# Softmax sums and reciprocals in two parts, with three changes of order in the layers after attention

## The chip, the cores and the metric

The kernel runs on one core of a Trainium2 chip. The metric is the device time of one execution in microseconds (us); the shown time is the median of three runs. All matrix products are made in fp32 accuracy: each operand is split into a high and a low part of type fp32r, and a product is three matmuls (high by high, high by low, low by high).

## The reference

Three layers follow each other. The first is attention in which a query sees only the keys with the same 6 sign bits (a hash by a random projection):

```python
def _attn_ref(q, k, v, proj):                       # q, k, v: 2 x 8 x 768 x 64
    q_bits = (einsum('bhsd,dk->bhsk', q, proj) > 0)  # proj: 64 x 6; k_bits the same
    mask = q_bucket[:, :, :, None] == k_bucket[:, :, None, :]
    scores = where(mask, scale * q @ k.T, -1e9)
    attn = exp(scores - max(scores))
    attn = attn / (sum(attn) + 1e-09)
    return attn @ v
def _moe_ref(x, w_gate, w_val, w_out):              # 1536 x 512 -> 1536 -> 512
    return (sigmoid(x @ w_gate) * (x @ w_val)) @ w_out
def _moe2_ref(x, w_in, w_out):                      # 1536 x 512 -> 2048 -> 512
    h = x @ w_in
    return where(h >= 1, h, where(h <= -1, 0, (h + 1) ** 2 / 4)) @ w_out
```

## The kernel before

The kernel is written by hand: one program for each engine, and semaphores between them. Each engine runs its own program strictly in order, so a wait holds up everything behind it on that engine.

**Attention** takes 96 steps g: 16 heads, and 6 blocks of 128 queries in each. Two heads make a pair i (g // 12), and u (g % 12) is the place in the pair. Three blocks make a half j (g // 3). A step has these pieces. TensorE (PE) makes the scores of block g (`scores`, L752 and L755). VectorE (DVE) reads them out of PSUM with the row minimum (`evacuate`, L1274). ScalarE (ACT) makes the exponential and its row sum (`exponential`, L979). GpSimd (POOL) multiplies the row by the reciprocal of its sum (`normalise`, L539). Five steps later PE transposes the probabilities (`turn_probs`, L764), ACT copies the high part (`high_probs`, L975), DVE makes the low part (`low_probs`, L1285), and PE multiplies by the values (`weigh`, L784 and L785).

Sums and reciprocals go by halves. POOL adds 1e-9 to three sums at once (`sums`, L534), DVE takes three reciprocals (`reciprocals`, L1279), and then POOL normalises the three blocks. In POOL's program stand between these: the splitting of the values of the next head in two instructions (`split_v`, L519 and L521) at u = 2 and u = 8, the sum of two output parts (`add_half`, L647), and in pairs 1 to 6, at u = 11, one part of the first weight set of the next layer (`first_set`, L552 to L559 and L588, L589).

PSUM has three double banks for scores, transposed probabilities and transposed inputs in turn: the use that comes three uses later may start only when the earlier one has been read out. For turn_probs(n) that is evacuate(n + 4). For scores(g) it is low_probs(g - 7), except where a transposition of queries or keys lies between; then it can be evacuate(g - 1). All engines count the same steps g. DVE's step is: hash bits (at two places of a pair), evacuate(g), reciprocals (every third step), low_probs(g - 5), low part of transposed queries or keys (at two places of a pair).

**The layers after attention** are 40 sets n of weights (24 for gate and value in turn, 16 for the last layer). They are multiplied by a scheme with 7 products for 8 blocks (`product(n, r)`, L806 to L808, 6 matmuls each), and the sums are formed while the products are read out of PSUM. ACT empties product 0 of a set (L1054) and DVE the six others (`empty`, L1342 and L1349). A product goes to one of the banks that `banks_for` names, and waits until what was last in that bank has been emptied. Sets 0, 12, 24 and 32 (`FIRSTS`) begin a new group of rows. Between products PE makes units of the output projection (`down`, L841 to L859); `units(n, r)` says how many after each product. On DVE, `value_set` multiplies the gates in: `gate_quarter` (L1362), `gate_second` (L1368) and `gate_first` (L1373). POOL forms sums of the weights and their low parts all the time (L552 to L577).

## Time and profile before

| | |
|---|---|
| median of 3 runs | 787.28 us (787.16 to 787.37) |
| the profiled execution | 787.15 us, its span 785.4 us |
| PE busy | 772.0 us, 98% of the span |
| DVE, ACT, POOL busy | 563.7, 461.1, 539.1 us |
| granted clock of PE, mean | 0.998 of full speed |

The trace is of one execution. A row of the timeline gives start, duration, engine, source line, operation, output<-inputs and the count of instructions that were put together; in brackets stands how long the engine was idle before it and what ended that. The starts of matmuls are measured and their ends are modelled; two matmuls of 384 columns that follow each other without a wait start 0.17 us apart.

### The profile page before, as it was taken

How to read it: one execution, taken by the hardware profiler on the slowest of the kernel's cores; microseconds unless marked ns; L12 is line 12 of the kernel's file. 1: busy time of each engine (PE TensorE's matmuls, PEld its weight loads, DVE VectorE, ACT ScalarE, POOL GpSimd, SP SyncE). 2: the span in 40 equal slices, each digit the busy share in tenths (PEclk: the TensorE clock that was granted, in tenths of full speed). 3: DMA queues.
4: the chain of work that ended last, by engine and by line, in shares of the span. 5: the costliest groups of instructions: out<-in, count | busy, mean ns of one | idle time of the engine just before them, and what ended most of it. 6: DMA issues, size and time to landing. Idle time of an engine off the chain costs nothing.

```text
span 785.4 us, 12212 instructions
## 1 busy us (share of the span) xinstructions
PE 772.0 (98%) x4403; PEld 717.3 (91%) x4403; DVE 563.7 (72%) x869; ACT 461.1 (59%) x731; POOL 539.1 (69%) x533
## 2 busy tenths in 40 slices
PE   7999999999999899999999999999999999999998
PEld 6899999999989899999899999999899988999996
DVE  6888888889888655665764666676777776756654
ACT  4889989989997442443463343356555475644433
POOL 4568667788889968877596877736957755565420
PEclk9999999999999999999999999999999999999999
DMA  7784675474300222122021221120121011201002
GB/s 153 181 189 107 164 164 114 101 165 108 92 1 12 71 81 75 34 81 81 28 82 55 67 68 40 68 81 28 56 80 54 29 52 52 84 28 53 1 1 81
DMA packets 61931, 60.09 MB, mean 77 GB/s; under 512 B 28384, under 2 KB 51632, under 8 KB 61872
## 3 DMA queue, kind: packets, MB, share of 16 engines
q1 hardware_dynamic: 61712, 59.32, 28.4%
q8 instruction: 35, 0.57, 0.3%
q14 instruction: 24, 0.20, 0.1%
q10 hardware_dynamic: 160, 0.00, 0.0%
HBM read 37.75 MB, written 3.15 MB: 52 GB/s over the span
## 4 chain that ended last, share of the span: by engine, by line
PE 86%; DVE 5%; ACT 4%; issue 3%; POOL 2%; DMA 0%; SPq 0%; DVEq 0%; POOLq 0%; ACTq 0%
PE ps L806 12%; PE ps L807 12%; PE ps L808 12%; PE ps L845 9%; PE ps L764 6%; PE ps L859 6%; PE ps L858 6%; PE ps L857 6%; PE ps L846 4%; PE ps L784 3%; PE ps L785 3%; PE ps L752 3%; PE ps L755 3%; ACT ph L975 1%; PE ps L713 1%
## 5 line engine op out<-in xcount | busy, mean ns | idle before, releaser
L806 PE MATMUL ps<-xop,wset 128*128 128x384 f32 x560 | 189.9, 339 | 2.6 <-DVE u L1349 2.1
L807 PE MATMUL ps<-xop,wset 128*128 128x384 f32 x560 | 189.1, 338 | 0.0
L808 PE MATMUL ps<-xop,wset 128*128 128x384 f32 x560 | 188.6, 337 | 0.0
L1349 DVE TENSOR_TENSOR u<-ps,u 128x384 f32<-128x384 f32 x144 | 79.7, 553 | 103.4 <-PE ps L808 102.6
L564 POOL TENSOR_TENSOR wset<-stage,wset 128x512 fp32r<-128x512 f32 x39 | 57.8, 1482 | 108.0 <-ACT wset L1022 108.0
L806 PEld LDWEIGHTS ps<-xop,wset 128*128 128x128 f32 x560 | 105.3, 188 | 13.1 <-DVE u L1349 3.2
L1285 DVE TENSOR_TENSOR pl<-ps,ph 128x768 fp32r<-128x768 f32 x96 | 91.6, 956 | 24.2 <-ACT ph L975 23.2
L807 PEld LDWEIGHTS ps<-xop,wset 128*128 128x128 f32 x560 | 105.4, 188 | 3.6
L539 POOL TENSOR_SCALAR probs<-probs,small 128x768 f32<-128x768 f32 x96 | 88.8, 932 | 24.6 <-DVE small L1279 21.9
L808 PEld LDWEIGHTS ps<-xop,wset 128*128 128x128 f32 x560 | 105.2, 188 | 0.0
L979 ACT ACTIVATE probs<-probs,small 128x768 f32<-128x768 f32 x96 | 90.0, 937 | 7.5 <-DVE probs L1274 6.9
L570 POOL TENSOR_TENSOR wset<-wsum,wset 128x1024 fp32r<-128x1024 f32 x39 | 94.3, 2418 | 0.0
L1274 DVE TENSOR_SCALAR_CACHE_REDUCE probs<-ps 128x768 f32<-128x768 f32 x96 | 90.9, 950 | 1.7 <-PE ps L755 1.1
L975 ACT CAST ph<-ps 128x768 fp32r<-128x768 f32 x96 | 76.8, 801 | 19.6 <-PE ps L764 17.8
L764 PE MATMUL ps<-ident,probs 128*128 128x128 f32 x576 | 79.0, 273 | 1.8 <-DVE probs L1274 1.6
L845 PE MATMUL ps<-hh,wo 128*128 128x512 f32 x192 | 75.5, 398 | 0.0
L764 PEld LDWEIGHTS ps<-ident,probs 128*128 128x128 f32 x576 | 67.3, 140 | 8.9 <-POOL probs L539 3.1
L859 PE MATMUL ps<-wo,hl 128*128 128x512 f32 x192 | 75.2, 392 | 0.0
L858 PE MATMUL ps<-wo,hh 128*128 128x512 f32 x192 | 75.2, 392 | 0.0
L857 PE MATMUL ps<-wo,hh 128*128 128x512 f32 x192 | 74.8, 389 | 0.0
L784 PE MATMUL ps<-ph,v 128*128 128x384 f32 x192 | 72.2, 376 | 0.1
L1054 ACT COPY u<-ps 128x384 f32<-128x384 f32 x40 | 19.1, 478 | 89.7 <-PE ps L808 89.6
(135 smaller groups left out, 1696.1 us busy)
## 6 DMA issues: line engine op xcount, KB each, us to landing
stage<-in_moe_w_in_dram SPq DMA_DIRECT2D x16, 512.0 KB, 3.9
stage<-in_moe_w_out_dram SPq DMA_DIRECT2D x14, 512.0 KB, 3.7
stage<-in_moe_w_gate_dram SPq DMA_DIRECT2D x12, 512.0 KB, 4.3
stage<-in_moe_w_val_dram SPq DMA_DIRECT2D x12, 512.0 KB, 3.6
ops<-qh SPq DMA_DIRECT2D x15, 384.0 KB, 5.2
ops<-kh SPq DMA_DIRECT2D x28, 192.0 KB, 3.4
qn<-in_q_dram SPq DMA_DIRECT2D x16, 192.0 KB, 4.5
kn<-in_k_dram SPq DMA_DIRECT2D x16, 192.0 KB, 4.3
```

The lines of the kernel that those rows point to most:

```text
L570: pool.tensor_tensor(weights(n, 1)[:, 3:7], wsum[:, :], weights(n, 0)[:, 3:7].bitcast(F32), ALU.subtract).then_inc(w_split, 1)
L764: last = pe.transpose(dst[:, t * P:(t + 1) * P], probs[n % RING][:, t * P:(t + 1) * P], ident[:, :])
L784: pe.matmul(o_bank(j), v2[h % 2][:, t, :], ph[j % 2][:, t, :], start=(t == 0), stop=False)
L806: pe.matmul(dst, high[:, c, :], high_x(r)[:, c, :], start=(c == 0), stop=False)
L807: pe.matmul(dst, high[:, c, :], low_x(r)[:, c, :], start=False, stop=False)
L808: last = pe.matmul(dst, low[:, c, :], high_x(r)[:, c, :], start=False, stop=(c == 1))
L845: pe.matmul(main, w[:, cols], h[:, t % 3, 0:512], start=(first and n == 0), stop=(last_tile and n == 2))
L857: pe.matmul(ps[:, r, :], hh[:, t % 3, rows], wh, start=first, stop=False)
L858: pe.matmul(ps[:, r, :], hh[:, t % 3, rows], wl, start=False, stop=False)
L859: last = pe.matmul(ps[:, r, :], hl[:, t % 3, rows], wh, start=False, stop=last_tile)
L1274: dve.tensor_scalar(probs[g % RING].rearrange("p (s n) -> p s n", s=2), score_slot(g), NO_MATCH, None, ALU.min, ALU.min, accum_out=lowest( ...
L1285: dve.tensor_tensor(pl[j % 2][:, :, cols], turned_slot("T", n).rearrange("p (t n) -> p t n", t=T), ph[j % 2][:, :, cols].bitcast(F32), ALU ...
```

## The change

Four things are changed.

1. Each half's sums and reciprocals are taken in two parts: blocks 0 and 1 of the half together (part 0), block 2 alone (part 1). POOL takes part 0 at its step g = 3j + 2 and part 1 at g = 3j + 3, and normalises block g - 2 instead of g - 3. DVE takes the reciprocals of part 0 at step 3j + 2 and of part 1 at 3j + 3, and behind low_probs instead of ahead of it.
2. The query bits of pair 1 are made at u = 7 instead of u = 6.
3. In sets 1 and 13, `gate_quarter` stands behind `empty(n, 2)` instead of behind `empty(n, 4)`.
4. Sets 25 and 33 have four banks instead of two for their first four products. In sets 11 and 23, one unit of the output projection is made after product 5 (11 instead of 12 are left for after product 6).

```diff
--- before.py
+++ after.py
@@ -159,7 +159,7 @@
             return (3, 6)[kind == "K"] if i else (5, 6)[kind == "K"]
 
         def bits_at(i, kind):
-            return signs_at(i, kind) + 1
+            return signs_at(i, kind) + 1 if i else 7
 
         uses = [("Q", 0), ("K", 0)]
         for g in range(STEPS):
@@ -228,6 +228,8 @@
             if n < 2:
                 return (4, 5, 2, 3) if n else (4, 5, 2) if r == R - 1 else (4, 5)
             if n in FIRSTS and r == R - 1 or n == FIRSTS[1] + 1 or n in (2, FIRSTS[1] + 2) and r < 2:
+                return (6, 7, 2, 3)
+            if n in (FIRSTS[2] + 1, FIRSTS[3] + 1) and r < 4:
                 return (6, 7, 2, 3)
             return (6, 7)
 
@@ -529,13 +531,14 @@
                     pool.wait_ge(coded[(i - 1) % 2][1], all_coded(i - 1, 1))
                 pool.tensor_scalar(codes[:, :], bits[:, :], mscale, 1.0, ALU.mult, ALU.mult).then_inc(z_codes, 1)
 
-            def sums(j):
-                pool.wait_ge(exp_done, HT * j + HT)
-                pool.tensor_scalar(total(HT * j, HT), total(HT * j, HT), EPS, 1.0, ALU.add,
-                                   ALU.mult).then_inc(sums_done, 1)
+            def sums(j, part):
+
+                n, m = HT * j + 2 * part, 2 - part
+                pool.wait_ge(exp_done, n + m)
+                pool.tensor_scalar(total(n, m), total(n, m), EPS, 1.0, ALU.add, ALU.mult).then_inc(sums_done, 1)
 
             def normalise(n):
-                pool.wait_ge(rcp_done, n // HT + 1)
+                pool.wait_ge(rcp_done, 2 * (n // HT) + 1 + n % HT // 2)
                 pool.tensor_scalar(probs[n % RING][:, :], probs[n % RING][:, :], rcp(n), 1.0, ALU.mult,
                                    ALU.mult).then_inc(normed, 1)
 
@@ -659,14 +662,16 @@
                     pool.wait_ge(z_codes, 1)
                 pool.tensor_copy(dst, src[D:P, :].bitcast(F32)).then_inc(second_keys, 1)
                 pool.wait_ge(second_keys, n + 1)
-            for g in range(STEPS + HT):
+            for g in range(STEPS + 2):
                 i, u = g // U, g % U
+                if g % HT == 2:
+                    sums(g // HT, 0)
                 if g % HT == 0 and g:
-                    sums(g // HT - 1)
-                if g >= HT:
-                    normalise(g - HT)
+                    sums(g // HT - 1, 1)
+                if g >= 2:
+                    normalise(g - 2)
                 if g % HT == 0 and 12 <= g < STEPS:
-                    add_half((g - 12) // HT, g - HT + 1)
+                    add_half((g - 12) // HT, g - 1)
                 if g < STEPS and g % T == 2:
                     split_v(g // T)
                 if u == bits_at(i, "K") and i < NP - 1:
@@ -882,7 +887,7 @@
                     return 0
                 if n < N1:
                     if ends:
-                        return 3 * KT if r == R - 1 else 0
+                        return {R - 2: 1, R - 1: 3 * KT - 1}.get(r, 0)
                     return int(r > 2 if n % 2 == 0 else r in (0, 1, 2, 4))
                 if ends:
                     return (2, 2, 1, 1, 1, 1, 20)[r]
@@ -1274,9 +1279,10 @@
                 dve.tensor_scalar(probs[g % RING].rearrange("p (s n) -> p s n", s=2), score_slot(g), NO_MATCH, None,
                                   ALU.min, ALU.min, accum_out=lowest(g)).then_inc(evacuated, 1)
 
-            def reciprocals(j):
-                dve.wait_ge(sums_done, j + 1)
-                dve.reciprocal(rcp(HT * j, HT), total(HT * j, HT)).then_inc(rcp_done, 1)
+            def reciprocals(j, part):
+                n, m = HT * j + 2 * part, 2 - part
+                dve.wait_ge(sums_done, 2 * j + part + 1)
+                dve.reciprocal(rcp(n, m), total(n, m)).then_inc(rcp_done, 1)
 
             def low_probs(n):
                 j = n // HT
@@ -1409,12 +1415,11 @@
                 t, g = 2 * pair_of(n), group_of(n) + 1
                 empty(n, 1)
                 empty(n, 2)
-                alone = n - 1 in FIRSTS or n + 1 in FIRSTS
-                if not alone:
+                if n + 1 not in FIRSTS:
                     gate_quarter(n)
                 empty(n, 3)
                 empty(n, 4)
-                if alone:
+                if n + 1 in FIRSTS:
 
                     gate_quarter(n)
                 empty(n, 5)
@@ -1490,10 +1495,12 @@
                 if u == bits_at(i, "K") and i < NP - 1:
                     make_bits(i + 1, True)
                 evacuate(g)
-                if g % HT == 0 and g:
-                    reciprocals(g // HT - 1)
                 if g >= LAG:
                     low_probs(g - LAG)
+                if g % HT == 2:
+                    reciprocals(g // HT, 0)
+                if g % HT == 0 and g:
+                    reciprocals(g // HT - 1, 1)
                 if i == NP - 1 and u in (4, 5):
                     rest_x(0, u - 4)
                 if u == turn_at(i, "Q") and i < NP - 1:
@@ -1501,7 +1508,7 @@
                 if u == turn_at(i, "K") and i < NP - 1:
                     low_turned("K", i + 1)
             rest_x(0, 4)
-            reciprocals(2 * NH - 1)
+            reciprocals(2 * NH - 1, 1)
             low_probs(STEPS - 5)
             low_probs(STEPS - 4)
             add_last(2 * NH - 3)
```

The source lines of the changed kernel are shifted by 2 to 6. In the order of instructions below, brackets name the semaphores that an instruction waits for.

POOL around steps 32 and 33 (u = 8 and 9 of a pair), the kernel before: L534 is `sums`, L539 `normalise`, L519 and L521 `split_v`, L647 `add_half`.

```order
L539 TENSOR_SCALAR probs<-probs,small 128x768 [waits rcp_done]
L519 CAST v<-vn 128x6x64 [waits o_ready,v_in0]
L521 TENSOR_TENSOR v<-vn,v 128x6x64 [waits v_high]
L534 TENSOR_SCALAR small<-small 128x3 [waits exp_done]
L539 TENSOR_SCALAR probs<-probs,small 128x768 [waits rcp_done]
L647 TENSOR_TENSOR x<-x,o_part 64x384 [waits o_copied,normed]
L539 TENSOR_SCALAR probs<-probs,small 128x768 [waits rcp_done,o_done]
L539 TENSOR_SCALAR probs<-probs,small 128x768 [waits rcp_done]
```

The same stretch of a pair in the changed kernel: `sums` is L538 there, `normalise` L542, `split_v` L521 and L523.

```order
L538 TENSOR_SCALAR small<-small 128x2 [waits exp_done]
L542 TENSOR_SCALAR probs<-probs,small 128x768 [waits rcp_done]
L521 CAST v<-vn 128x6x64 [waits o_ready,v_in1]
L523 TENSOR_TENSOR v<-vn,v 128x6x64 [waits v_high]
L538 TENSOR_SCALAR small<-small 128x1 [waits exp_done]
L542 TENSOR_SCALAR probs<-probs,small 128x768 [waits rcp_done]
L650 TENSOR_TENSOR x<-x,o_part 64x384 [waits o_copied,normed]
L542 TENSOR_SCALAR probs<-probs,small 128x768 [waits rcp_done,o_done]
```

The two instructions of `split_v` stood ahead of the sums of three blocks; now they stand between the two parts, behind the normalisation of the half's first block.

DVE over three steps of a pair, the kernel before: L1274 is `evacuate`, L1279 `reciprocals`, L1285 `low_probs`.

```order
L1274 TENSOR_SCALAR probs,small<-ps 128x768 [waits pt_ready,scores_ready]
L1285 TENSOR_TENSOR pl<-ps,ph 128x6x128 [waits pt_high]
L1274 TENSOR_SCALAR probs,small<-ps 128x768 [waits pt_ready,scores_ready]
L1279 RECIPROCAL small<-small 128x3 [waits sums_done]
L1285 TENSOR_TENSOR pl<-ps,ph 128x6x128 [waits pt_high]
L1274 TENSOR_SCALAR probs,small<-ps 128x768 [waits pt_ready,scores_ready]
```

And in the changed kernel, with `evacuate` at L1279, `reciprocals` at L1285 and `low_probs` at L1291:

```order
L1279 TENSOR_SCALAR probs,small<-ps 128x768 [waits pt_ready,scores_ready]
L1291 TENSOR_TENSOR pl<-ps,ph 128x6x128 [waits pt_high]
L1285 RECIPROCAL small<-small 128x2 [waits sums_done]
L1279 TENSOR_SCALAR probs,small<-ps 128x768 [waits pt_ready,scores_ready]
L1291 TENSOR_TENSOR pl<-ps,ph 128x6x128 [waits pt_high]
L1285 RECIPROCAL small<-small 128x1 [waits sums_done]
```

There are now two reciprocals, one behind each of two successive steps of DVE, and each waits for its own sums.

## Rows read from the trace of the kernel before

**Rows 1.** Page, part 1: busy time of each engine, share of the span, instructions.
```profile
PE 772.0 (98%) x4403; PEld 717.3 (91%) x4403; DVE 563.7 (72%) x869; ACT 461.1 (59%) x731; POOL 539.1 (69%) x533
```

**Rows 2.** Windows: stretch and length; busy time of PE, PEld, DVE, ACT, POOL; granted clock; DMA.
```profile
210.00:260.00 50.00, 48.64 (x299) 44.70 (x299) 41.34 (x71) 40.89 (x69) 44.20 (x48) 1.00 0.07 22
267.30:270.60 3.30, 3.30 (x11) 2.51 (x11) 2.25 (x4) 0.90 (x1) 3.22 (x3) 0.51 0.69 245
```

**Rows 3.** Timeline, DVE, steps 32 to 34 (start, duration, line, operation, idle before).
```profile
88.35 0.95 DVE L1274 TENSOR_SCALAR_CACHE_REDUCE probs<-ps 128x768 f32<-128x768 f32 x1
...
89.22 0.17 DVE L1279 RECIPROCAL small<-small 128x3 f32<-128x3 f32 x1
89.72 0.96 DVE L1285 TENSOR_TENSOR pl<-ps,ph 128x768 fp32r<-128x768 f32 x1 [0.33 <-ACT ph L975]
90.60 0.95 DVE L1274 TENSOR_SCALAR_CACHE_REDUCE probs<-ps 128x768 f32<-128x768 f32 x1
```

**Rows 4.** Timeline, POOL, a split of the values and what follows, without idle.
```profile
216.26 0.49 POOL L519 CAST v<-vn 128x384 fp32r<-128x384 f32 x1
216.84 1.01 POOL L521 TENSOR_TENSOR v<-vn,v 128x384 fp32r<-128x384 f32 x1
217.94 0.20 POOL L534 TENSOR_SCALAR small<-small 128x3 f32<-128x3 f32 x1
218.44 0.91 POOL L539 TENSOR_SCALAR probs<-probs,small 128x768 f32<-128x768 f32 x1 [0.30 <-DVE small L1279]
```

**Rows 5.** Timeline, DVE, the reciprocal between the last two rows above.
```profile
218.18 0.18 DVE L1279 RECIPROCAL small<-small 128x3 f32<-128x3 f32 x1
```

**Rows 6.** Timeline, PE, transposition of block 30 in step 35 (u = 11).
```profile
91.89 0.82 PE L764 MATMUL ps<-ident,probs 128*128 128x128 f32 x6
```

**Rows 7.** Timeline, DVE, steps 27 and 28 (u = 3 and 4).
```profile
73.12 0.95 DVE L1274 TENSOR_SCALAR_CACHE_REDUCE probs<-ps 128x768 f32<-128x768 f32 x1
...
74.22 0.96 DVE L1285 TENSOR_TENSOR pl<-ps,ph 128x768 fp32r<-128x768 f32 x1
...
75.75 0.96 DVE L1274 TENSOR_SCALAR_CACHE_REDUCE probs<-ps 128x768 f32<-128x768 f32 x1
```

**Rows 8.** Timeline, PE, scores of step 29 (u = 5).
```profile
77.56 0.51 PE L752 MATMUL ps<-ops 128*128 128x384 f32 x2
```

**Rows 9.** Timeline, POOL, the first part of the first weight set (u = 11, pair 1).
```profile
64.59 0.74 POOL L552 TENSOR_TENSOR wsum<-stage 128x256 f32<-128x256 f32 x1
...
66.81 0.20 POOL L534 TENSOR_SCALAR small<-small 128x3 f32<-128x3 f32 x1
```

**Rows 10.** Timeline, DVE, evacuations of steps 24 and 25 (u = 0 and 1).
```profile
66.07 0.95 DVE L1274 TENSOR_SCALAR_CACHE_REDUCE probs<-ps 128x768 f32<-128x768 f32 x1
...
68.06 0.95 DVE L1274 TENSOR_SCALAR_CACHE_REDUCE probs<-ps 128x768 f32<-128x768 f32 x1
```

**Rows 11.** Timeline, DVE, set 1's first gating, and the emptying that PE waits for.
```profile
259.97 2.10 DVE L1362 TENSOR_TENSOR hid<-hid,u 128x384 f32<-128x384 f32 x1
...
265.71 0.56 DVE L1349 TENSOR_TENSOR u<-ps,u 128x384 f32<-128x384 f32 x1
```

**Rows 12.** Timeline, POOL, weight set 2 beside it.
```profile
257.31 1.29 POOL L564 TENSOR_TENSOR wset<-stage,wset 128x512 fp32r<-128x512 f32 x1
...
259.25 2.41 POOL L570 TENSOR_TENSOR wset<-wsum,wset 128x1024 fp32r<-128x1024 f32 x1
```

**Rows 13.** Timeline, PE, product 3 of set 2.
```profile
266.33 0.44 PE L806 MATMUL ps<-xop,wset 128*128 128x384 f32 x1 [2.13 <-DVE u L1349]
```

**Rows 14.** Timeline, PE, sets 11 and 33: last matmul before a short gap, first behind it.
```profile
376.46 0.34 PE L808 MATMUL ps<-xop,wset 128*128 128x384 f32 x1
376.87 0.44 PE L806 MATMUL ps<-xop,wset 128*128 128x384 f32 x1
...
665.85 0.34 PE L808 MATMUL ps<-xop,wset 128*128 128x384 f32 x1
666.41 0.44 PE L806 MATMUL ps<-xop,wset 128*128 128x384 f32 x1 [0.22 <-ACT u L1054]
```

## The prediction

> **What bounds the kernel now.** I read the page's first part first: PE is busy 98% of the span [rows 1], so little can be won, and anything that holds PE up is paid in full. The windows say where PE still waits. Between 210 and 260 us, the last pair of heads and the change to the next layer, it is busy 48.64 of 50 us, and in a stretch of 3.3 us behind the largest wait its granted clock is 0.51 of full speed, the lower of its two levels, 1.2 GHz [rows 2]. Then I read the timelines of DVE and PE side by side, because in attention DVE follows PE closely. The reader is to see that nothing separates the instructions of DVE at steps 33 and 34: low_probs starts at 89.72 and lasts some 0.87 us to the next start, and evacuate(34) starts at 90.60 at once [rows 3]. That evacuation lasts about 0.95 us with the read of its accumulator, and PE can start about 0.15 us later, so turn_probs(30) could start at 91.71. It starts at 91.89 [rows 6]. DVE has 0.18 us to spare there.
>
> **Part 1, the sums and reciprocals.** What it removes is nothing: the same three blocks are summed, inverted and normalised. What it adds are 32 more sums of 0.20 us on POOL and 32 more reciprocals, of which each holds DVE for 0.09 us. What it moves is the point: the reciprocal of part 1 waits on DVE for a sum that POOL makes only after it has normalised the first block, and after that block has waited for part 0's reciprocal, which DVE makes one step earlier. So between two successive steps of DVE, POOL now has a chain of its own, and what is queued behind the waiting reciprocal on DVE is evacuate(3j + 4), for which PE and ACT wait.
>
> The price of that chain comes from POOL's rows. From a reciprocal to the normalisation behind it pass 0.26 us, from a sum to the reciprocal 0.24 us, a split of the values lasts 0.58 + 1.10 us to the sum behind it, and a normalisation 0.87 us [rows 4, 5]. From DVE's one reciprocal to the end of its next (0.09 us) the chain is 0.27 + 0.87 + 1.69 + 0.24 + 0.09 = 3.16 us with a split, 1.47 us without one, and 3.7 us with the 2.22 us of the first weight set's first part [rows 9].
>
> At u = 8 DVE reaches part 0's reciprocal at 88.35 and would reach part 1's at 90.60, 2.25 us later [rows 3]. It must wait until 91.51: evacuate(34) is 0.91 us late, and with 0.18 us to spare turn_probs(30) is 0.73 us late. The six middle pairs (1 to 6) have this pattern with 0.70 to 0.75 us; pair 0 gives 0.34 and pair 7 0.58 by the same working. Together 4.4 + 0.9 = **5.3 us**.
>
> At u = 2 part 0 is at 73.12, and low_probs ends at 75.09, where the hash bits follow and then, at 75.75, evacuate(28) [rows 7]. The chain ends at 76.28, and bits and evacuation are 1.18 us late. The scores of step 29 wait for that evacuation; they start at 77.56 [rows 8], 0.70 us after it would let them (75.75 + 1.11 = 76.86). The stall is 0.47 us, six times, and 0.44 in pair 7, which is 3.3 us. In pair 0 part 1 holds up the low part of the keys and all that follows until step 7. No row shows this wait; its bounds are 0, if the values' split is done in time, and the chain's full delay of 1.2 us. I take 0.9, nearer to the upper end, since DVE does not wait for PE in those steps. Together **4.2 us**.
>
> At u = 11 of pairs 1 to 6 a part of the first weight set stands in the place of the split: 1.3 to 2.25 us, the longest in pair 1 [rows 9]. There evacuate(25) started at 68.06 and part 0 is at 66.07 [rows 10]; the chain ends at 69.79, the delay is 1.73 us, the reserve 0.50 us and the stall 1.24 us. The other five give 0.34, 0.93, 0.47, 0.99 and 0.51. Together **4.5 us**. At u = 5 nothing stands on POOL between the parts; 1.47 us is less than DVE's own two instructions, and the cost is nothing. If POOL came late there, it would cost what u = 8 does.
>
> What part 1 gives: blocks are normalised up to one step earlier. In the steady pairs turn_probs starts where the evacuation lets it, 0.18 us later, and not where POOL lets it [rows 3, 6], so that is worth nothing. In the last pair and at the start PE waits for evacuations and not for POOL, and I take nothing for it there either; the most it could give is a part of the 1.4 us that PE idles between 210 and 260 us [rows 2].
>
> **Part 2, the query bits.** They are 0.5 us of DVE moved from ahead of evacuate(6) to ahead of evacuate(7), for which turn_probs(3) waits at once. The work ahead of evacuate(7) stays the same, so it gives nothing.
>
> **Part 3, the gating.** In set 1 gate_quarter takes 2.10 us instead of some 0.5, and ends when POOL's L570 has ended and half a microsecond more has passed: 259.97 + 2.10 = 262.07 against 259.25 + 2.41 = 261.66 [rows 11, 12]. Placed behind empty(n, 2), it would be reached at 257.5, inside L564, which ends at 258.6 [rows 12], and be done at 259.0. But the products in between are emptied by 261.0, and then gate_second, with two inputs in SBUF as well, comes before POOL's long L570 is over, which by now is 0.45 us later itself. It would run from 262.1, the last gating would be done near 264.7, and the empty(2, 1) that PE waits for starts at 264.8 instead of 265.71 [rows 11]. The wait of 2.13 us [rows 13] shrinks by **0.85 us**. The Trainium skill (SBUF — State Buffer, Who interferes with whom) says that a DVE instruction with two SBUF inputs and a GpSimd instruction that reads SBUF shut each other out for the whole instruction and don't share the time; by this rule the moved gate only hands the block on to the next one. If they shared the bandwidth, the move would give up to 1.5 us, and the sum below would be 0.65 us lower. The trace agrees with the rule: the 2.10 us end 0.41 us after L570.
> In set 13 the same move ends PE's short wait for the first hidden tile, 0.45 us. The clock: PE ran at the lower level for 3.3 us [rows 2] from about 1 us after its wait; that cost 1.7 us. Whether 1.3 us of waiting does it too no row tells; I leave the 1.7 us in, and put them into the range.
>
> **Part 4, banks and units.** The gaps before products in sets 11 and 33 are 0.24 and 0.38 us over the regular 0.17, with 0.11 us more behind each [rows 14]; sets 23 and 25 have the like, 0.34 and 0.39 us. All four waits are for a bank, and go. The unit that moves is PE work moved to where PE waited; what it covered after product 6 has 11 units left. Together **1.6 us**.
>
> **The sum.** 5.3 + 4.2 + 4.5 = 14.0 us are lost, 0.85 + 0.45 + 1.6 = 2.9 us are won: 11.1 us more than the profiled execution's 787.15 us (0.13 below the median of the three), and so 798.2 us.
>
> **The rivals.** *POOL is in time.* If DVE in the new order reaches part 1's reciprocal 3.2 us after part 0's and not 2.25, nothing waits, and what is left are parts 3 and 4: 787.3 - 2.9 = 784.4 us, or 782.7 us if the clock stays up. This is the faster side. It decides at u = 8: whether the two steps of DVE are longer than POOL's chain. For it speaks that DVE is idle 0.33 and more before low_probs [rows 3], so it has air in some steps; against it, that this idle time is already in the 2.25 us.
> *Half is absorbed.* A late DVE need not hold PE if PE is late itself: once the pair has lost its 0.7 us at u = 8, the stalls at u = 11 and u = 2 may find more reserve. Then only u = 8, the start and half of the rest count: 5.3 + 0.9 + 3.9 - 2.9 = 7.2, and less if u = 2 goes wholly: 791 to 794.5 us.
> *The delays go through whole.* DVE is busy without a gap at u = 8 to 11, and ACT with it. If the reserves are gone after the first delay, each costs its full length: 6.8 at u = 8, 8.4 at u = 2 and the start, 7.0 at u = 11, less 2.9: 19 us more, 806 us.
> *The change doesn't do what it says:* the blocks are normalised earlier, and no instruction of PE starts earlier for it. This is part of my forecast, not against it.
>
> **Chances.** The forecast (794.5 to 802 us) 0.58, half absorbed (789 to 794.5) 0.15, whole delays (802 to 807) 0.13, POOL in time 0.10, and 0.04 that gains and losses meet near zero. The range of 8 in 10 leaves out the faster case and the far end of the whole delays: 790.5 to 804 us. Faster by over 0.2% (1.6 us, about what a measurement of this kernel can tell from no change) 0.09, within it 0.04, slower 0.87.
>
> **What would show it.** In the changed kernel DVE's reciprocals have 20 or so waits for POOL's sums of 0.5 to 1.7 us, at u = 3, 9 and 0 of the pairs; PE's waits for evacuations by DVE grow from under 2 us to over 8; the last pair ends near 254 instead of 240 us. PE's wait in set 2 is 1.3 us instead of 2.13, and those in sets 11, 23, 25 and 33 are gone. I am wrong if the reciprocals of part 1 run without idle time before them, or if they wait and the transpositions behind don't move.

## The result, and the profile after

The changed kernel takes **799.5 us** (median of 4 runs, 799.2 to 799.9), the kernel before 787.22 us beside it (785.75 to 787.37): 1.0161 times as long, with a 95% interval of 1.0147 to 1.0175. Slower was forecast, 798.2 us in a range of 790.5 to 804.0. The profiled execution took 799.71 us, its span is 797.6 us, 12.2 us more than before.

The page of the changed kernel, its part 1 and, below, the shares of the chain that ended last:

```profile
PE 776.8 (97%) x4403; PEld 716.1 (90%) x4403; DVE 564.5 (71%) x901; ACT 462.2 (58%) x731; POOL 544.0 (68%) x565
```

```profile
PE 76%; POOL 7%; issue 7%; DVE 6%; ACT 3%; DMA 0%; SPq 0%; POOLq 0%; DVEq 0%; ACTq 0%
```

DVE's busy time grew by 0.8 us for 32 more reciprocals, POOL's by 4.9 us for 32 more sums (compare [rows 1]); no work that was added explains 12 us. The chain now runs 7% of its length through POOL, an engine that is idle for a third of the time. The waits of the changed kernel show how (engine, what waits, line, releaser; us in all, times, longest):

```profile
POOL probs L542 <- DVE small L1285: 44.7, 32, 2.2
...
DVE small L1285 <- POOL small L538: 19.2, 24, 1.5
...
PE ps L769 <- DVE probs L1279: 6.8, 12, 1.2
...
PE ps L757 <- DVE probs L1279: 2.0, 3, 0.9
```

L1285 is `reciprocals`, L538 `sums`, L542 `normalise`, L1279 `evacuate`; L769 is the transposition `turn_probs` and L757 `scores`. POOL waits for DVE's reciprocal and DVE for POOL's sum, in turn: each engine has air, and neither can use it. The row for the wait of DVE's reciprocals was 1.5 us in 4 waits before, and it is 19.2 us in 24 waits now. The third and fourth rows are what PE pays of it.

Now one place in full, u = 8 of pair 2, where [rows 3] and [rows 6] stood before. Timeline of DVE in the changed kernel:

```profile
93.42 0.15 DVE L1285 RECIPROCAL small<-small 128x2 f32<-128x2 f32 x1
93.49 0.94 DVE L1279 TENSOR_SCALAR_CACHE_REDUCE probs<-ps 128x768 f32<-128x768 f32 x1
...
94.79 0.96 DVE L1291 TENSOR_TENSOR pl<-ps,ph 128x768 fp32r<-128x768 f32 x1 [0.36 <-ACT ph L980]
96.44 0.16 DVE L1285 RECIPROCAL small<-small 128x1 f32<-128x1 f32 x1 [0.69 <-POOL small L538]
96.54 0.96 DVE L1279 TENSOR_SCALAR_CACHE_REDUCE probs<-ps 128x768 f32<-128x768 f32 x1
```

Timeline of POOL beside it, which does without a gap what DVE waits for:

```profile
93.67 0.91 POOL L542 TENSOR_SCALAR probs<-probs,small 128x768 f32<-128x768 f32 x1 [2.19 <-DVE small L1285]
94.52 0.50 POOL L521 CAST v<-vn 128x384 fp32r<-128x384 f32 x1
95.11 1.02 POOL L523 TENSOR_TENSOR v<-vn,v 128x384 fp32r<-128x384 f32 x1
96.22 0.19 POOL L538 TENSOR_SCALAR small<-small 128x1 f32<-128x1 f32 x1
```

And PE, the scores of step 35 and the transposition of block 30, which waits for evacuate(34):

```profile
96.26 0.51 PE L757 MATMUL ps<-ops 128*128 128x384 f32 x2
...
97.65 0.84 PE L769 MATMUL ps<-ident,probs 128*128 128x128 f32 x6 [0.54 <-DVE probs L1279]
```

From the one reciprocal to the end of the next pass 96.44 + 0.09 - 93.42 = 3.11 us. DVE's own work between them would have ended 0.69 us earlier. The transposition starts 1.39 us after the scores, where it was 0.69 us before: 0.70 us lost. In the other middle pairs (1 to 6) it is 0.66 to 0.71 us at this place, and 0.12 to 0.13 us more at the first scores of the next pair.

The table gives the length of each pair (from its first scores to the next pair's, the last one to the transposition of block 95), from the starts in the traces of the kernel before, the changed one, and three experiments that are told below:

| pair | before | changed | lost | part 1 alone (e1) | split later (e3) | both later (e4) |
|---|---|---|---|---|---|---|
| 0 | 23.17 | 24.56 | 1.39 | 25.47 | 23.21 | 23.23 |
| 1 | 28.65 | 30.02 | 1.37 | 30.04 | 28.67 | 28.62 |
| 2 | 28.74 | 31.20 | 2.46 | 31.24 | 30.21 | 28.87 |
| 3 | 28.76 | 30.40 | 1.64 | 30.40 | 29.43 | 28.85 |
| 4 | 28.79 | 30.71 | 1.92 | 30.72 | 29.75 | 28.87 |
| 5 | 28.79 | 30.36 | 1.57 | 30.43 | 29.42 | 28.86 |
| 6 | 28.77 | 30.94 | 2.17 | 30.92 | 29.95 | 28.86 |
| 7 | 37.09 | 39.36 | 2.27 | 39.41 | 39.99 | 39.03 |

Attention lost 14.8 us. The layers behind it won 3.3 us. The first scores came at 13.47 instead of 12.80 us, 0.7 us later, and the three make the 12.2 us. This start varies: over all traces of this case it lies between 12.79 and 14.58 us. PE's first transpositions, in the kernel before and in the changed one:

```profile
5.10 0.88 PE L713 MATMUL ps<-ident,qn 128*128 128x128 f32 x6 [0.38 <-DMA qn<-in_q_dram]
```

```profile
5.07 1.54 PE L718 MATMUL ps<-ident,qn 128*128 128x128 f32 x6 [0.30 <-DMA qn<-in_q_dram]
```

The queries were there as early as before; the six transpositions took 1.54 us instead of 0.88, with a granted clock of 1.00 shown in both traces. Why is open. In e3 and e9 below, which have part 1 too, the scores start at 12.99 and 13.18 us. So the 0.7 us are not put down to the change.

Behind attention PE's large wait ahead of product 3 of set 2 has become short. Timeline of PE (before: [rows 13]), and of the gating and POOL's L573 ahead of it (before: [rows 11, 12]), in the changed kernel:

```profile
280.62 0.45 PE L811 MATMUL ps<-xop,wset 128*128 128x384 f32 x1 [0.72 <-DVE u L1355]
```

```profile
273.09 1.44 DVE L1368 TENSOR_TENSOR hid<-hid,u 128x384 f32<-128x384 f32 x1
...
276.62 1.68 DVE L1374 TENSOR_TENSOR hid<-hid,tmp 128x768 f32<-128x768 f32 x1
```

```profile
275.08 2.40 POOL L573 TENSOR_TENSOR wset<-wsum,wset 128x1024 fp32r<-128x1024 f32 x1
```

The wait is 0.72 us instead of 2.13, and the granted clock did not fall behind it.

### The profile page after: what moved, and what is told of

Same layout as the page of the kernel before. It is cut to its first block, busy times and chain, and to the rows that moved or that the text cites. A ratio compares the mean times of both kernels' runs of the same rounds, so it can differ in the third digit from the quotient of the medians.

```text
span 797.6 us, 12278 instructions
## 1 busy us (share of the span) xinstructions
PE 776.8 (97%) x4403; PEld 716.1 (90%) x4403; DVE 564.5 (71%) x901; ACT 462.2 (58%) x731; POOL 544.0 (68%) x565
## 4 chain that ended last, share of the span: by engine, by line
PE 76%; POOL 7%; issue 7%; DVE 6%; ACT 3%; DMA 0%; SPq 0%; POOLq 0%; DVEq 0%; ACTq 0%
PE ps L811 11%; PE ps L812 11%; PE ps L813 11%; PE ps L850 8%; PE ps L862 6%; PE ps L864 6%; PE ps L863 6%; PE ps L851 4%; PE ps L769 4%; POOL probs L542 3%; PE ps L757 2%; PE ps L760 2%; PE ps L789 2%; PE ps L790 1%; ACT ph L980 1%
## 5 line engine op out<-in xcount | busy, mean ns | idle before, releaser
L542 POOL TENSOR_SCALAR probs<-probs,small 128x768 f32<-128x768 f32 x96 | 88.9, 927 | 50.3 <-DVE small L1285 44.7
L1291 DVE TENSOR_TENSOR pl<-ps,ph 128x768 fp32r<-128x768 f32 x96 | 91.6, 955 | 21.4 <-ACT ph L980 19.1
L573 POOL TENSOR_TENSOR wset<-wsum,wset 128x1024 fp32r<-128x1024 f32 x39 | 94.3, 2417 | 0.0
L1279 DVE TENSOR_SCALAR_CACHE_REDUCE probs<-ps 128x768 f32<-128x768 f32 x96 | 90.7, 947 | 1.3 <-PE ps L760 1.1
L769 PE MATMUL ps<-ident,probs 128*128 128x128 f32 x576 | 79.3, 274 | 8.7 <-DVE probs L1279 6.8
L769 PEld LDWEIGHTS ps<-ident,probs 128*128 128x128 f32 x576 | 66.1, 140 | 19.6 <-POOL probs L542 11.9
L1355 DVE TENSOR_TENSOR hid<-ps,u 128x384 f32<-128x384 f32 x84 | 46.5, 554 | 35.4 <-PE ps L813 33.8
```

Of the source, the lines that this page charges most:

```text
L542: pool.tensor_scalar(probs[n % RING][:, :], probs[n % RING][:, :], rcp(n), 1.0, ALU.mult, ALU.mult).then_inc(normed, 1)
L573: pool.tensor_tensor(weights(n, 1)[:, 3:7], wsum[:, :], weights(n, 0)[:, 3:7].bitcast(F32), ALU.subtract).then_inc(w_split, 1)
L769: last = pe.transpose(dst[:, t * P:(t + 1) * P], probs[n % RING][:, t * P:(t + 1) * P], ident[:, :])
L1291: dve.tensor_tensor(pl[j % 2][:, :, cols], turned_slot("T", n).rearrange("p (t n) -> p t n", t=T), ph[j % 2][:, :, cols].bitcast(F32), ALU ...
L1355: dve.tensor_tensor(dst, bank(n, r), other, ALU.add).then_inc(e_dve, 1)
```

## The experiments

The first question was whether part 1 alone makes the loss, and whether the rest is worth what was said.

**e1_parts_alone** is the kernel before with part 1 and nothing else.

> The kernel before with part 1 of the change alone (sums and reciprocals of each half in two parts), the other three parts undone. Theory (the reciprocal of part 1 waits on DVE for a sum that stands behind the split of the values or a part of the first weight set on POOL): all of the loss is here, 14 to 15 us, so 801 to 802.5 us. Rival (the loss of 12.3 us is shared between attention and the changes behind it, some of which cost): below 799.5 us.

Measured: 803.0 us (802.47 to 803.78), 1.0198 [1.0179, 1.0218]. The pairs from 1 on are as long as in the changed kernel (table), and the waits are the same:

```profile
DVE small L1283 <- POOL small L536: 19.4, 24, 1.5
```

That is 15.6 us more than the kernel before beside it (787.45), 0.5 us above the forecast of 801 to 802.5. So the whole loss is part 1's. Pair 0 is 0.9 us longer than in the changed kernel. That has a cause of its own: with part 1, PE waits at the start twice for about 1 us (before the change once), and in this trace (windows: stretch, length, busy PE, PEld, DVE, ACT, POOL, clock) the clock fell behind it, while in the changed kernel's it did not:

```profile
22.50:26.00 3.50, 3.50 (x16) 3.47 (x15) 2.43 (x6) 2.53 (x5) 0.94 (x2) 0.59 1.08 219
```

```profile
22.50:26.00 3.50, 3.50 (x25) 3.46 (x24) 2.60 (x7) 3.28 (x6) 0.74 (x3) 1.00 1.07 224
```

In the same stretch PE issued 16 matmuls at 0.59 of full speed, and 25 in the changed kernel. The mean clock was 0.998 in all four runs of e1, and 1.0 in all four of the changed kernel.

**e2_without_parts** is the changed kernel without part 1, so parts 2 to 4 on the kernel before.

> The changed kernel with part 1 undone: only the gating, the banks and units and the query bits are changed. Theory: 3.3 us less than before (set 2's wait and the stretch at the lower clock behind it go, and four short waits for banks), 783.9 us. Rival (the clock's stretch went by chance of the run, and only waits are won): 2 us less or fewer, 785.3 us or more.

Measured: 783.99 us (783.88 to 785.57), 0.9961 [0.9948, 0.9973]: 3.5 us less than the kernel before beside it (787.45), and the fastest kernel of this study. Its attention is as long as before (232.69 us to block 95, 232.76 before). The gains behind attention are real and stand beside part 1's loss; they don't come from it.

The second question was what in part 1 costs the time. The theory names POOL's instructions between the two parts. Their place can be changed without taking any work away.

**e3_split_later**: the values are split one step later, behind the second sum.

```diff
                     sums(g // HT - 1, 1)
+                if g < STEPS and g % T == 3:
+                    split_v(g // T)
                 if g >= 2:
                     normalise(g - 2)
...
-                if g < STEPS and g % T == 2:
-                    split_v(g // T)
```

> The changed kernel with one thing moved on POOL: the split of the values stands right behind the sum of part 1 (at u = 3 and 9) instead of ahead of it (u = 2 and 8). Same instructions, same number of waits. Theory: the waits at the start, at u = 3 and at u = 9 go, 9.5 us of the loss, so 790 us; what is left are the parts of the first weight set, 4.5 us. Rival (the many small instructions and round trips between POOL and DVE cost the time wherever the split stands): 797 to 800 us.

Measured: 792.46 us (791.98 to 792.69), 1.0063 [1.0045, 1.0081], 7.0 us less than the changed kernel; 9.5 us less had been expected, so the size was missed. Pair 1, whose only POOL work between parts was the split, is back at 28.67 us. Pairs 2 to 6 are still too long by 1.47, 0.67, 0.96, 0.63 and 1.18 us, which follow the lengths of the first weight set's parts in the order that the forecast had (1.24, 0.34, 0.93, 0.47 and 0.99), 0.03 to 0.33 us larger. And the last pair is 2.90 us too long, more than in the changed kernel. The place, in step 24 of this kernel, POOL and then DVE:

```profile
66.64 0.91 POOL L542 TENSOR_SCALAR probs<-probs,small 128x768 f32<-128x768 f32 x1 [0.41 <-DVE small L1285]
67.51 0.74 POOL L555 TENSOR_TENSOR wsum<-stage 128x256 f32<-128x256 f32 x1
68.21 0.74 POOL L556 TENSOR_TENSOR wsum<-stage 128x256 f32<-128x256 f32 x1
68.89 0.74 POOL L558 TENSOR_TENSOR wsum<-wsum,stage 128x256 f32<-128x256 f32 x1
69.72 0.19 POOL L538 TENSOR_SCALAR small<-small 128x1 f32<-128x1 f32 x1
```

```profile
66.39 0.15 DVE L1285 RECIPROCAL small<-small 128x2 f32<-128x2 f32 x1
...
69.95 0.16 DVE L1285 RECIPROCAL small<-small 128x1 f32<-128x1 f32 x1 [1.49 <-POOL small L538]
```

From part 0 to the end of part 1 pass 3.65 us; 3.7 had been worked out.

**e4_both_moved**: besides, the first weight set's parts stand at u = 0 of the next pair, behind the second sum.

```diff
+                if u == 0 and 2 <= i < 8:
+                    first_set(i - 2)
...
-                if 1 <= i < 7 and u == 11:
-                    first_set(i - 1)
```

> As the run before, and the parts of the first weight set stand behind the sum of part 1 too (u = 0 of the next pair instead of u = 11). Theory: no reciprocal waits long for POOL any more, another 4.5 us go, 785 to 786 us, within 2 us of the kernel without part 1. Rival (round trips): 796 us or more.

Measured: 787.16 us (786.75 to 788.94), 0.9999 [0.9987, 1.0011], 1 to 2 us above what was expected. Pairs 1 to 6 have 28.62 to 28.87 us, as before the change, and the waits of DVE's reciprocals shrank:

```profile
DVE small L1284 <- POOL small L538: 3.4, 6, 1.1
```

With the same 64 sums and 64 reciprocals, 12.3 us of the changed kernel's time are gone. So the count of instructions costs next to nothing; without the work that stands on POOL between the two parts there is no loss in the middle pairs. That blocks are normalised earlier brings nothing either: the pairs are not shorter than before. What is left against e2 is 3.2 us by the medians and 4.2 us by the traces: 1.7 us of a late start in this kernel's trace (14.58 us against 12.91), 1.9 us in the last pair (39.03 against 37.09), and 0.5 us in the others. In the last pair 0.8 us are lost at the transposition of block 80, where PE waits for an evacuation (in e3 too, and not in the changed kernel), and 1.0 us at that of block 95.

**e8_one_more and e9_two_more** ask for the threshold: to e4 they add one or two instructions on POOL between the parts at u = 5 of pairs 1 to 6, where nothing stood. They add up `ident` into a tile that no one reads; the second kernel has `range(2)`.

```diff
+                if u == 5 and 1 <= i < 7:
+                    for m in range(1):
...
+                        pool.tensor_tensor(spare.rearrange("p (a n) -> p a n", a=3),
+                                           ident.rearrange("p (a n) -> p a n", a=1).to_broadcast([P, 3, P]),
+                                           ident.rearrange("p (a n) -> p a n", a=1).to_broadcast([P, 3, P]),
+                                           ALU.add).then_inc(spared, 1)
```

> The kernel of run e4 (787.2 us) with one additional instruction of some 1.0 us on POOL between the two parts at u = 5 of pairs 1 to 6, which no one uses; it adds work and changes no result. Theory (the chain between the parts grows from 1.47 to 2.5 us, DVE comes after 2.25 us, and PE has 0.4 us to spare): within 0.5 us of e4, 787.2 to 787.7 us. Rival (each further microsecond on POOL costs, since POOL is loaded): 6 us more, 793 us.

> As the run before with two such instructions, 2.2 us. Theory: the chain is 3.7 us against 2.25, DVE waits 1.4 to 1.5 us and PE 1.0 to 1.1 us in each of six pairs: 6 to 6.6 us more than e4, 793.5 us, and all of it with the second instruction. Rival (proportional to POOL's load): twice what the first one cost.

Measured: 788.06 us (787.84 to 788.69), 1.0013 [1.0002, 1.0023], and 793.34 us (793.22 to 793.52), 1.0079 [1.0058, 1.0100]. The first instruction, six times, costs 0.9 us, where up to 0.5 had been expected, the second one 5.3 us. This refutes the rival by which the second costs as much as the first. One of them holds POOL for 0.87 us. With two, POOL and DVE at step 29:

```profile
83.64 1.73 POOL L685 TENSOR_TENSOR rest<-ident 128x384 f32<-128x384 f32 x2
85.46 0.19 POOL L538 TENSOR_SCALAR small<-small 128x1 f32<-128x1 f32 x1
```

```profile
85.69 0.16 DVE L1292 RECIPROCAL small<-small 128x1 f32<-128x1 f32 x1 [0.85 <-POOL small L538]
```

The chain is 1.47 us without an instruction in it, 2.34 with one and 3.21 with two, against 2.25 us between DVE's steps. So by this sum it is late by 0.1 us with one, which PE's reserve of 0.18 us should take up, and by 1.0 us with two. With one, pairs 1, 3 and 4 are 0.04 to 0.06 us longer than in e4, and pairs 2, 5 and 6 0.3 to 0.4 us. In pairs 5 and 6 DVE waits in that trace for the sum of part 0 at u = 5 (0.25 and 0.22 us) and then for that of part 1 (0.29 and 0.26 us); in pairs 1 to 4 it waits for neither, and what pair 2 loses is open. Work on an engine that is idle for 30% of the time was nearly free up to a certain length, and cost its full length from there.

**e10_reciprocal_first** changes DVE's order and leaves POOL's: in the changed kernel the reciprocals stand again ahead of `low_probs`.

```diff
                 evacuate(g)
-                if g >= LAG:
-                    low_probs(g - LAG)
                 if g % HT == 2:
                     reciprocals(g // HT, 0)
                 if g % HT == 0 and g:
                     reciprocals(g // HT - 1, 1)
+                if g >= LAG:
+                    low_probs(g - LAG)
```

> The changed kernel with the reciprocals ahead of low_probs on DVE, as they stood before, still in two parts. Theory: the distance between the two reciprocals stays 2.2 us and POOL's chain 3.2 us, but DVE's own wait of 0.3 to 0.5 us for the high part now lies behind the reciprocal and takes up some of the delay: 2 to 4 us less, 795.5 to 797.5 us. Rival (the place behind low_probs is what costs): 788 us or less. A third (the place on DVE matters not at all): 799.5 us.

Measured: 792.37 us (790.86 to 792.46), 1.0063 [1.0044, 1.0082]. It is 7.1 us less than the changed kernel, where 2 to 4 us had been expected: a miss on the size, and the measured time lies between the theory's and the rival's (788 us or less). The trace shows why, at the same u = 8. DVE:

```profile
91.52 0.16 DVE L1285 RECIPROCAL small<-small 128x2 f32<-128x2 f32 x1
...
94.55 0.16 DVE L1285 RECIPROCAL small<-small 128x1 f32<-128x1 f32 x1 [0.72 <-POOL small L538]
94.63 0.94 DVE L1291 TENSOR_TENSOR pl<-ps,ph 128x768 fp32r<-128x768 f32 x1
95.49 0.95 DVE L1279 TENSOR_SCALAR_CACHE_REDUCE probs<-ps 128x768 f32<-128x768 f32 x1
```

The reciprocal waits as long as before, 0.72 us. But `low_probs` behind it has lost its own wait for ACT, 0.36 us in the changed kernel: the two waits now lie side by side and not one behind the other. PE pays less for it:

```profile
95.71 0.53 PE L757 MATMUL ps<-ops 128*128 128x384 f32 x2
...
96.59 0.85 PE L769 MATMUL ps<-ident,probs 128*128 128x128 f32 x6
```

That is 0.88 us after the scores, with 0.69 before the change and 1.39 in the changed kernel; at u = 2 nothing is lost at all. Over all, DVE still waits 17.9 us for POOL's sums, hardly less than 19.2, and PE's wait for the transposition's bank is down from 6.8 to 2.2 us:

```profile
DVE small L1285 <- POOL small L538: 17.9, 27, 1.1
...
PE ps L769 <- DVE probs L1279: 2.2, 3, 1.0
```

So by the times nearly half of part 1's loss (7.1 of 15.5 us, the changed kernel against e2) hangs on the second half of the edit, the place of the reciprocals behind `low_probs` and directly ahead of `evacuate`. By the traces it is more. In this one the clock fell at the start, as in e1, and pair 0 has 25.79 us, 1.2 more than in the changed kernel:

```profile
22.50:26.00 3.50, 3.50 (x17) 3.47 (x16) 2.01 (x5) 2.64 (x5) 1.79 (x4) 0.62 1.09 222
```

In pairs 1 to 7 the order takes away 8.2 of the 13.4 us. The two halves don't add up: with POOL's work moved (e4) the same place costs nothing in the middle pairs, so the loss takes both, a chain that is too long and a place where nothing hides it. The forecast had counted the two together and never asked what each did.

**e11_tail** looks at what e4 left in the last pair: the last reciprocal stands behind low_probs(91) and (92).

```diff
             rest_x(0, 4)
-            reciprocals(2 * NH - 1, 1)
             low_probs(STEPS - 5)
             low_probs(STEPS - 4)
+            reciprocals(2 * NH - 1, 1)
```

> The kernel with the values' split and the first weight set's parts moved behind the second sums (787.2 us), and with one more change: the last reciprocal, of block 95, stands on DVE behind the low parts of blocks 91 and 92 and not ahead of them. In the trace it waits 1.08 us for POOL's last sum while low_probs(91), for which PE waits, is behind it. Expected: low_probs(91) and (92) come about 1 us earlier, normalise(95) later, but PE needs block 95 last: about 1 us less, 786.2 us. Rival: the end of attention is set by the normalisation of blocks 93 to 95 on POOL, and nothing is gained or up to 0.5 us is lost.

Measured: 786.36 us (785.98 to 788.0), 0.9989 [0.9976, 1.0003], 0.8 us less than e4 by the medians, which is within the spread of the two; in the traces the last pair has 37.97 us instead of 39.03, with 37.09 before. The wait that it took away is in the changed kernel too, and the stall of PE that comes of it, at the transposition of block 95:

```profile
255.22 0.16 DVE L1285 RECIPROCAL small<-small 128x1 f32<-128x1 f32 x1 [1.08 <-POOL small L538]
```

```profile
261.02 0.74 PE L769 MATMUL ps<-ident,probs 128*128 128x128 f32 x5 [0.60 <-DVE pl L1291]
```

The third question was how the 3.3 us of the other parts divide.

**e5_gate_alone** is the kernel before with part 3 alone.

```diff
-                alone = n - 1 in FIRSTS or n + 1 in FIRSTS
-                if not alone:
+                if n + 1 not in FIRSTS:
                     gate_quarter(n)
...
-                if alone:
+                if n + 1 in FIRSTS:
```

> The kernel before with the moved gate_quarter alone (sets 1 and 13). Theory (set 2's wait shrinks from 2.1 to 0.7 us and the granted clock then stays at the upper level): 1.4 + 0.45 + 1.7 us less, 783.8 us, and no stretch at the lower clock. Rival (the clock's stretch stays or comes elsewhere, only the waits go): 785.5 us.

Measured: 785.22 us (784.56 to 786.63), 0.9977 [0.9967, 0.9987], 2.1 us less, where 3.5 had been expected. The time is nearer to the rival's (785.5), but in the trace the clock stays up as the theory has it. The theory had taken the clock's fall for part of every run of the kernel before; 13 of the 23 runs beside e5 have a mean clock below 1.0. An estimate from this: 1.3 us of waits, and 1.4 us of clock in 13 of 23 runs, are 2.1 us.

**e6_banks_units** is part 4 alone, and **e7_bits_alone** part 2 alone.

> The kernel before with part 4 alone: four banks for the first products of sets 25 and 33, and one unit of the output projection after product 5 in sets 11 and 23. The prediction's term is 1.6 us: the gaps in sets 11, 23, 25 and 33 go and nothing new comes, 785.7 us where the kernel before has 787.3. A rival from the trace of the changed kernel, where small new gaps stand near sets 3, 12, 13 and 33: half of it comes back as other waits, 786.5 us. The kernels with all of parts 2 to 4 (3.3 us less) and with the gate alone (2.1 us less) leave 1.2 to 1.3 us for this part.

> The kernel before with part 2 alone: the query bits of pair 1 at u = 7. The prediction's term is 0: 787.3 us, and turn_probs(3) 0.5 us later against turn_probs(2) 0.5 us earlier, with the same time from step 12 on. Rival: the bits stood ahead of an evacuation for which PE waited, and stand now where nothing waits: 0.4 to 0.5 us less, 786.8 us.

Measured: e6 786.79 us (785.39 to 788.61), 0.9996 [0.9984, 1.0008]; e7 787.46 us (786.1 to 788.01), 0.9995 [0.9983, 1.0007]; the kernel before had 787.68 us beside them. Neither can be told from no change by its time, and e6 is nearer to its rival's 786.5 us than to the 785.7 of the prediction's term. The starts of the sets in the traces tell more, since they leave out what varies elsewhere. The first product of a set, against the kernel before (us):

| set | e5, gate | e6, banks, units | e7, bits | changed |
|---|---|---|---|---|
| 2 | -0.08 | -0.07 | -0.04 | +15.47 |
| 3 | -2.83 | +0.12 | -1.40 | +12.75 |
| 5 | -2.56 | +0.14 | -1.40 | +13.02 |
| 12 | -2.56 | +0.10 | -1.40 | +12.85 |
| 15 | -2.75 | +0.13 | -1.37 | +12.71 |
| 24 | -2.54 | +0.01 | -1.16 | +12.58 |
| 26 | -2.54 | -0.20 | -1.10 | +12.42 |
| 34 | -2.54 | -0.42 | -1.08 | +12.19 |

The bits do nothing up to set 2. Banks and units win 0.12 us in set 23, and 0.2 in each of sets 25 and 33, together 0.55 us. Against e1, e5 and e7, which have the same code as the kernel before in these sets but take 0.21 us longer in set 23, it is 0.76 to 0.87 us. In set 11 they win nothing, since the unit that was moved leaves a gap later. In e6 it is this one, behind the units after product 6:

```profile
381.90 0.28 PE L848 MATMUL ps<-hh,wo 128*128 128x256 f32 x1
382.34 0.50 PE L847 MATMUL ps<-hh,wo 128*128 128x512 f32 x1 [0.17 <-DVE hl L1355]
```

And e7, which changes nothing there, is 1.4 us ahead behind set 2. The windows of the same stretch as in [rows 2] say why:

```profile
267.30:270.60 3.30, 3.21 (x18) 2.69 (x17) 2.47 (x5) 0.92 (x1) 3.22 (x3) 1.00 0.63 215
```

PE had waited 2.13 us as in the kernel before, and the clock stayed up. Of the 29 runs of the kernel before beside e6, 12 have a mean granted clock of 1.0, with spans around 784.5 us, and 17 one below it, with spans around 786.0 us. The median of the kernel before holds this fall, that of a kernel without the large wait doesn't: in the traces of e2 and e5 the clock doesn't fall there, and 18 of their 19 runs have a mean of 1.0.

## Why the prediction was right, and where it was off

**The mechanism** was right, and so was its place. The sizes fit by the pair; by the place they fit less well. The chain between the reciprocals is 3.11 us (forecast 3.16) with a split and 3.65 us (3.7) with the longest of the first weight set's parts. The gap of PE at the u = 8 shown is 0.70 us (0.70 to 0.75). Pairs 1 to 6 lost 11.1 us, 1.37, 2.46, 1.64, 1.92, 1.57 and 2.17; the forecast's terms for the same stretches are 1.16, 2.46, 1.55, 2.14, 1.67 and 2.20, 11.2 us. Pair 0 lost 1.39 us (1.24).

That the pairs fit so well is in part luck. The starts in the traces, step by step, give 0.78 to 0.84 us for u = 8, with what it costs the next pair's first scores (0.73 was forecast), 1.42, 0.64, 0.90, 0.59 and 1.13 us for the parts of the first weight set (1.24, 0.34, 0.93, 0.47 and 0.99), and for u = 2 only 0.18 us in pairs 2 to 6 (0.47). Pair 1 lost 0.37 us at u = 2, and 0.31 at step 14, which no term had. The term for u = 2 was mis-sized: it had the scores of step 29 stall, and in pair 2 they start 1.00 us behind the late evacuation, at no loss; only the transposition behind them is late, by 0.18 us. What was too much there made up for what was too little at the other two.

**What it said would show** did: 24 waits of DVE's reciprocals of up to 1.5 us, PE's waits for evacuations at 6.8 + 2.0 us, the first product of the next layer at 254.74 instead of 240.04 us. Two signs came otherwise: the wait in set 2 is 0.72 us and not 1.3, and of the waits in sets 11, 25 and 33 a part came back elsewhere (Part 4).

**The last pair** is the term that was too small: 2.27 us against 0.58 + 0.44 + 0.51 = 1.53. The step that failed looked at the three places that a pair has, and at the end of attention only asked what part 1 could give. There the last reciprocal waits 1.08 us for a sum behind a normalisation that takes 1.5 us instead of 0.9, with low_probs(91) queued behind it; PE lost 0.76 us at the transposition of block 95. e11 took that wait away.

**Part 3** was forecast at 0.85 + 0.45 us, with the clock's 1.7 us kept in the forecast as still lost. In e5 set 3 starts 2.83 us earlier. 1.4 of it are the clock, by e7, and the rest, 1.4, the wait, which shrank from 2.13 to 0.70 us. The forecast had `gate_second` last past POOL's L570 and the last gating done near 264.7; both came 0.3 to 0.4 us earlier, the end of `gate_second` at 262.7 and that of the last gating at 264.3. Some was given back in set 4 (0.27 us), 0.18 won in set 14 and not 0.45. So 1.1 to 1.3 us without the clock, which is about the sum of the forecast, from terms that were each off by 0.3: 1.1 us in place of 0.85, and 0.18 in place of 0.45.

**The clock** was the choice with the least behind it: 1.7 us left in. Such a fall costs 1.4 us, and the clock stayed up in all four runs of the changed kernel. The forecast had put this into its range and not into its middle. Here too luck helped: without these 1.4 us the layers behind attention would have won 1.9 us and not 3.3, against a forecast of 2.9.

**Part 4** was forecast at 1.6 us and gave 0.55 to 0.87. The step took each gap that would go as won, and for the unit said that what it covered had enough left. In set 11 a gap of the same size opened behind it; in sets 25 and 33 some 0.2 us came back further on, at the output units; in set 23 the gap went. **Part 2** was forecast at nothing, and e7 has nothing.

In sum, part 1 and the late start 15.5 instead of 14.0, the rest 3.3 instead of 2.9: 12.2 instead of 11.1 us.

**The rivals.** That POOL is in time fell with the 24 waits. That half is absorbed fell for u = 8 and u = 11, whose losses e3 and e4 take away one after the other; for u = 2 of pairs 2 to 6 it holds, since 0.3 of the 0.47 us were absorbed. That the delays go through whole fell too: at u = 8 the evacuation starts 0.88 us after low_probs lets go of DVE (94.79 + 0.87 to 96.54), and PE lost 0.70 of it at once; the reserve of 0.18 us was there in each middle pair. And that the earlier normalisation is worth nothing holds: e4, which has it without the waits, is not faster in any pair than the kernel before.

**What the forecast did not see** is e10. Part 1 is two edits, a chain on POOL, and the move of the reciprocals from ahead of a wait to behind it. It named the first and priced both together. The sum came out, with half of the reason.

## What to carry to other kernels

Where two engines hand small results to and fro, write down the time of one round (here 1.47 us for a sum, a reciprocal and a normalisation) and the distance between the two places in the waiting engine's program (2.25 us): what the other engine does in between was nearly free up to the difference, and was paid in full past it, however idle both engines look in the busy shares. If an instruction must wait for another engine, put it directly ahead of one that waits anyway, not behind that one and ahead of what the busiest engine needs. And test an edit that has several parts part by part: here three small ones were worth some 3.3 us, and the large one hid them.

## What the runs showed of the hardware

**The clock does not follow the wait alone.** Behind the same wait of 2.13 us it fell to 0.51 for 3.3 us in the kernel before [rows 2] and stayed at 1.00 in e7; in the kernel before it fell in 17 of 29 runs by their means. Such a fall cost 1.4 us. With part 1 there is a second place, the start, where two waits of 1 us with 1.8 us of work between them came before a fall in e1 (0.59 over 3.5 us) and e10 (0.62), and before none in the trace of the changed kernel. What decides it is open. A saving that removes such a wait is worth more than the wait, on the average of many runs.

**POOL and DVE exclude each other.** The gating, with two inputs in SBUF, was started in the changed kernel at 273.09 beside this one, and ended at 274.53, 0.42 us after it:

```profile
272.82 1.29 POOL L567 TENSOR_TENSOR wset<-stage,wset 128x512 fp32r<-128x512 f32 x1
```

In the kernel before it ended 0.41 us after another one that it had met [rows 11, 12]. The other way round a normalisation, which lasts 0.91 us, takes 1.54 us when a DVE instruction with two inputs in SBUF is under way. In the changed kernel:

```profile
253.20 0.94 DVE L1302 TENSOR_TENSOR xop<-early,xop 128x768 fp32r<-128x768 f32 x1
```

```profile
253.38 1.54 POOL L542 TENSOR_SCALAR probs<-probs,small 128x768 f32<-128x768 f32 x1 [0.50 <-DVE small L1285]
```

It begins 0.18 us into the DVE instruction and ends 0.78 us after it. Over all traces of this case 26 normalisations begin within such a DVE instruction, 0.18 to 0.67 us into it; they last 1.49 to 1.62 us, and each ends 0.77 to 0.79 us after the DVE instruction, wherever it had begun. Two engines that shared the time would not give one and the same distance. This agrees with what the Trainium skill (SBUF — State Buffer, Who interferes with whom) says of the two engines, that whichever issues first holds the ports for its whole instruction. But which is first can't be read off the starts in a trace: six normalisations start 0.13 to 0.24 us ahead of such a DVE instruction, and still end 0.78 us after it, while the DVE instruction takes its usual 0.94 us. One that starts 0.68 us ahead takes its 0.91 us. The forecast had used the rule for the gating only; it holds for the normalisation too, and at the end of attention that delay was on the path.
